# Sliding-window attention scores as fp32 matmuls of raw queries and keys in alternate halves of the array

## What is computed

```python
def _attn_ref(q, k, v, n_sink, window):          # n_sink = 4, window = 128
    scores = np.matmul(q, k.transpose(0, 1, 3, 2)) / np.sqrt(D)
    rel = pos[:, None] - pos[None, :]
    keep = (pos[None, :] < n_sink) | ((rel >= 0) & (rel < window))
    a = softmax(np.where(keep, scores, -1e9))
    return np.matmul(a, v)
x = attn_out.transpose(0, 2, 1, 3).reshape(B, S, H * D)
x = _moe_ref(x, ...)    # 4 experts of causal attention (head of 64), two chosen per token
return _moe2_ref(x, ...)  # x + gated(gelu(x @ w_in)) @ w_out with a mixing of tokens
```

## Time and profile before

| | us |
|---|---|
| median of 3 runs | 470.83 |
| lowest and highest run | 469.19 and 471.52 |
| profiled execution, span from first to last instruction | 465.9 |
| stage 1 in it, scores from 10.4, last sinks weighed | 143.8 |
| TensorE busy | 427.5 (92%) |
| VectorE busy | 281.2 (60%) |
| ScalarE busy | 209.7 (45%) |
| GpSimd busy | 127.9 (27%) |

### The profile page before, as it was taken

How to read it: one execution, slowest core, us unless ns; L and a number is a source line. 1 busy time by engine, 2 the same in 40 slices (tenths; PEclk the granted TensorE clock), 3 DMA queues, 4 the chain that set the end, 5 groups by cost and what they waited for, 6 DMA issues and landing times.

```text
span 465.9 us, 8125 instructions
## 1 busy us (share of the span) xinstructions
PE 427.5 (92%) x2608; PEld 383.6 (82%) x2608; DVE 281.2 (60%) x703; ACT 209.7 (45%) x529; POOL 127.9 (27%) x144
## 2 busy tenths in 40 slices
PE   1897978779799999998999899899999999999997
PEld 1787968779699999997999799788888888888885
DVE  1889698896985778555177965347633235552322
ACT  2666566655663666554476555343311013330100
POOL 7765375455627600000003820034100000000000
PEclk9888699886999999999999999999999999999999
DMA  8755554743323300000001320010000110000011
GB/s 209 167 145 133 144 146 102 172 103 105 100 85 114 113 1 2 2 0 1 1 0 40 97 69 1 0 47 0 1 0 24 45 46 24 0 1 0 24 45 68
DMA packets 14157, 27.73 MB, mean 60 GB/s; under 512 B 2256, under 2 KB 5328, under 8 KB 14128
## 3 DMA queue, kind: packets, MB, share of 16 engines
q1 hardware_dynamic: 14128, 27.35, 21.8%
HBM read 24.20 MB, written 3.15 MB: 59 GB/s over the span
## 4 chain that ended last, share of the span: by engine, by line
PE 77%; DVE 10%; issue 8%; ACT 2%; DVEq 1%; DMA 1%; POOL 1%; SPq 0%; ACTq 0%; POOLq 0%
PE banks L825 12%; PE banks L827 12%; PE banks L826 12%; PE banks L1097 11%; PE banks L999 6%; PE banks L876 6%; PE banks L977 4%; PE banks L840 4%; PE banks L988 4%; PE banks L856 2%; DVE sinks L567 2%; DVE SM L552 2%; DVE RI L585 1%; PE banks L891 1%; PE banks L945 1%
## 5 line engine op out<-in xcount | busy, mean ns | idle before, releaser
L401 ACT ACTIVATE Pa<-SM,NM 128x260 f32<-128x260 f32 (+1 forms) x96 | 47.1, 491 | 36.5 <-DVE NM L552 36.4
L876 PE MATMUL banks<-va,PTa 128*128 128x64 f32 x352 | 52.5, 299 | 0.0
L876 PEld LDWEIGHTS banks<-va,PTa 128*128 128x128 f32 x352 | 51.9, 224 | 0.0
L552 DVE CUSTOM_DVE_ANT_0 SM<-banks,win 128x260 f32<-128x260 f32 (+1 forms) x96 | 37.9, 404 | 19.9 <-PE banks L840 13.9
L840 PE MATMUL banks<-kS,qH 128*128 128x260 f32 x96 | 38.2, 402 | 11.5 <-POOL qL L321 10.4
L999 PE MATMUL banks<-vg,PTb 128*128 128x64 f32 x336 | 44.6, 267 | 0.7 <-DVE Y L678 0.7
L999 PEld LDWEIGHTS banks<-vg,PTb 128*128 128x128 f32 x336 | 42.2, 191 | 1.6 <-issue 0.9
L458 ACT ACTIVATE Pb<-Pb,NM 128x128 f32<-128x128 f32 (+5 forms) x48 | 31.9, 665 | 21.4 <-DVE NM L664 21.3
L825 PE MATMUL banks<-w_inH,x2H 128*128 128x512 f32 x96 | 38.1, 397 | 0.0
L527 ACT ACTIVATE gH<-banks 128x512 fp32r<-128x512 f32 x12 | 7.2, 600 | 68.4 <-PE banks L1117 68.4
L827 PE MATMUL banks<-w_inH,x2L 128*128 128x512 f32 x96 | 37.5, 391 | 0.0
(11 more groups left out here) (150 smaller groups left out, 1118.0 us busy)
## 6 DMA issues: line engine op xcount, KB each, us to landing
kd<-in_kT SPq DMA_DIRECT2D x32, 198.0 KB, 3.6
qd<-in_qT SPq DMA_DIRECT2D x32, 192.0 KB, 3.8
va<-in_v SPq DMA_DIRECT2D x16, 192.0 KB, 3.4
out<-O SPq DMA_DIRECT2D x12, 256.0 KB, 2.0
raw<-in_w_sgT SPq DMA_DIRECT2D x9, 256.0 KB, 2.7
raw<-in_w_in SPq DMA_DIRECT2D x8, 256.0 KB, 2.6
raw<-in_w_b SPq DMA_DIRECT2D x8, 193.0 KB, 3.7
raw<-in_w_out SPq DMA_DIRECT2D x4, 256.0 KB, 2.9
```

The costliest lines, as they stand in the source:

```text
L401: nc.scalar.activation(Pa[s][:, t, a:WIN], SM[t % RING][:, a:WIN], ACT.Exp, bias=NM[:, s, t:t + 1], scale=-1.0, accum_out=RS[:, s, t:t + 1 ...
L552: nc.vector.tensor_tensor_reduce(out=SM[t % RING][:, a:WIN], in0=banks[:, A_BANKS[t % RING], 0:WIN - a], in1=m[:, :], scale=-SCALE, scalar ...
L876: last = nc.tensor.matmul(banks[:, 6 + s, t * D:(t + 1) * D], PTa[m][:, j * P:(j + 1) * P], va[s][:, t - 1 + own, :], start=(t == 0), stop ...
```

## The change

Queries and keys are no longer split: `split_queries`, `high_keys` and `low_keys` go, with their calls and the semaphores `q_split`, `k_high` and `k_split`. One fp32 matmul of the raw `qd` and `kd` makes a tile of scores. It has the 64 features as rows; even tiles take partitions 0 to 63 of `qd` and `kd`, and so the array's lower 64 rows, odd tiles 64 to 127. The two tiles of a pair are issued one behind the other, at turns 0, 2 and 4. `load_keys` now waits until head - 2 has been scored. A tile named `spare` keeps the place of the removed buffers. The transfers and their order stay.

```diff
-            qH, qL = [sb(f"qH{s}", [P, S], F32R, st) for s in range(2)], [sb(f"qL{s}", [P, S], F32R, st) for s in range(2)]
-            kS = [sb(f"kS{s}", [P, KEXT], F32R, st) for s in range(2)]
+            sb("spare", [P, 4 * S + 2 * KEXT], F32, st)
...
             def load_keys(s, head, again):
 
                 if again:
-                    sp.wait_ge(s_["q_split"], 2 * (head - 1))
-                    sp.wait_ge(s_["k_split"], head - 1)
+                    sp.wait_ge(s_["scored"], T * (head - 1))
...
-            def split_queries(s, head, turn, again):
-                pool.wait_ge(qk_in[s], 64 * (turn + 1))
-                if again:
-                    pool.wait_ge(s_["scored"], T * (head - 1))
-                pool.sem_inc(s_["pool_tick"], 1)
-                nc.gpsimd.tensor_scalar(qH[s][:, :], qd[s][:, :], 1.0, 0.0, ALU.mult, ALU.add).then_inc(s_["q_split"], 1)
-                pool.wait_ge(s_["q_split"], 2 * head + 1)
-                nc.gpsimd.tensor_tensor(qL[s][:, :], qd[s][:, :], qH[s][:, :].bitcast(F32), ALU.subtract)\
-                    .then_inc(s_["q_split"], 1)
...
-            def high_keys(s, head, turn, again):
-                act.wait_ge(qk_in[s], 64 * (turn + 1))
-                if again:
-                    act.wait_ge(s_["scored"], T * (head - 1))
-                nc.scalar.activation(kS[s][:, :], kd[s][:, :], ACT.Copy).then_inc(s_["k_high"], 1)
...
-            def low_keys(s, head):
-                dve.wait_ge(s_["k_high"], head + 1)
-                half = slice(D, P)
-                nc.vector.tensor_tensor(kS[s][half, :], kd[s][half, :], kS[s][half, :].bitcast(F32), ALU.subtract)\
-                    .then_inc(s_["k_split"], 1)
...
-            def score_tile(s, head, t, again):
+            def score_tile(s, head, t, turn, again):
 
                 if t == 0:
-                    pe.wait_ge(s_["q_split"], 2 * head + 2)
-                    pe.wait_ge(s_["k_split"], head + 1)
+                    pe.wait_ge(qk_in[s], 64 * (turn + 1))
                 if again or t >= RING:
                     pe.wait_ge(s_["masked"], T * head + t - RING + 1)
                 c = 0 if t == 0 else (t - 1) * BLK + SINK
-                for q, first_ in ((qH, True), (qL, False)):
-                    last = nc.tensor.matmul(banks[:, A_BANKS[t % RING], 0:WIN], q[s][:, t * P:(t + 1) * P], kS[s][:, c:c + WIN],
-                                            start=first_, stop=not first_)
-                last.then_inc(s_["scored"], 1)
+                half = slice(t % 2 * D, (t % 2 + 1) * D)
+                nc.tensor.matmul(banks[:, A_BANKS[t % RING], 0:WIN], qd[s][half, t * P:(t + 1) * P], kd[s][half, c:c + WIN],
+                                 start=True, stop=True).then_inc(s_["scored"], 1)
...
                 for t in range(T):
                     if nxt:
-                        score_tile(1 - s, head + 1, t, True)
+                        if t % 2 == 0:
+                            score_tile(1 - s, head + 1, t, turn + s, True)
+                            score_tile(1 - s, head + 1, t + 1, turn + s, True)
```

More of the change, by code:

```diff
@@ L184, in fused_attention_experts_gated @@
             "consts", "pool_step",
-            "q_split", "k_high", "k_split", "scored", "masked", "expd", "turned", "turned_in_act", "turned_in_dve",
+            "scored", "masked", "expd", "turned", "turned_in_act", "turned_in_dve",
             "sinks_gathered", "sinks_turned", "sinks_high", "sinks_in", "sv_in", "sv_high", "sv_low", "vs_ready",
@@ L338, in lay_out_sinks @@
                                         diag[:, :].unsqueeze(2).broadcast_to((SROWS, T, D)), ALU.mult).then_inc(s_["vs_ready"], 1)
-            for s in range(2):
-                split_queries(s, s, 0, False)
             split_strip(0, slice(0, WB_STEP))
@@ L346, in _ @@
             with pool.Fori(1, PAIRS) as i:
-                split_queries(0, 2 * i, i, True)
                 lay_out_sinks(0, 2 * i, True)
-                split_queries(1, 2 * i + 1, i, True)
                 split_strip(i, bass.ds(i * WB_STEP, WB_STEP))
@@ L415, in x_high, with act_step @@
                                      ACT.Copy).then_inc(s_["x_high"], 1)
-            def act_step(s, head, again, keys, nxt):
+            def act_step(s, head, again, nxt):
                 copy_group(s, head, 0, again)
@@ L424, in act_step @@
                         x_high(0, t)
-                    if t == 0 and keys is not None:
-                        high_keys(s, head + 2, keys, True)
                     if t == 2:
                         copy_group(s, head, 2, again)
-            high_keys(0, 0, 0, False)
-            high_keys(1, 1, 0, False)
             for t in range(T):
@@ L436, in _ @@
                 exp_tile(0, 0, t, False)
-            act_step(0, 0, False, 1, True)
-            act_step(1, 1, True, 1, True)
+            act_step(0, 0, False, True)
+            act_step(1, 1, True, True)
             with act.Fori(1, PAIRS - 1) as i:
[L440 to L443, removed]
+                act_step(0, 2 * i, True, True)
+                act_step(1, 2 * i + 1, True, True)
+            act_step(0, HEADS - 2, True, True)
+            act_step(1, HEADS - 1, True, False)
             def wait(name, n):
@@ L603, in x_low, with dve_step @@
                                         xH[:, :, t * P:(t + 1) * P].bitcast(F32), ALU.subtract).then_inc(s_["x_low"], 1)
-            def dve_step(s, head, before, again, keys, nxt):
+            def dve_step(s, head, before, again, nxt):
                 for t in range(T):
@@ L616, in dve_step @@
                         copy_group(s, head, again)
-                    if t == 2 and keys:
-                        low_keys(s, head + 2)
                     if t == 3:
@@ L623, in dve_step @@
                 invert_sums(s, head, again)
-            low_keys(0, 0)
-            low_keys(1, 1)
             for t in range(T):
@@ L631, in _ @@
             nc.vector.tensor_tensor(sv[low, :], sv_raw[low, :], sv[low, :].bitcast(F32), ALU.subtract).then_inc(s_["sv_low"], 1)
-            dve_step(0, 0, None, False, True, True)
-            dve_step(1, 1, 0, True, True, True)
+            dve_step(0, 0, None, False, True)
+            dve_step(1, 1, 0, True, True)
             with dve.Fori(1, PAIRS - 1) as i:
[L635 to L638, removed]
+                dve_step(0, 2 * i, i - 1, True, True)
+                dve_step(1, 2 * i + 1, i, True, True)
+            dve_step(0, HEADS - 2, PAIRS - 2, True, True)
+            dve_step(1, HEADS - 1, PAIRS - 1, True, False)
             normalise(1, HEADS - 1, PAIRS - 1)
@@ L921, in _ @@
             for t in range(T):
-                score_tile(0, 0, t, False)
+                score_tile(0, 0, t, 0, False)
             pe_step(0, 0, 0, False, True)
```

## The result

The changed kernel takes 478.7 us (median of 4 runs, 478.04 to 480.17) against 470.02 for the kernel before (4 runs beside it); the ratio is 1.0175, with a 95% interval of 1.0131 to 1.0219. So the change makes the kernel slower, by 8.7 us. The forecast was 472.0 in a range of 460 to 485, with 0.38 on slower by over 0.5%; the time that came is that of rival 3, 479, and not that of the central sum.

The account below looks back on a forecast made before the run. Stage 1 was taken as bound by TensorE's work plus a splitting stall, replaced by a wait for values. Start -1.5, steps 0 and 1 -1.4, loop +1.6, step 14 +1.0, half clock +1.5: +1.2 in all, 472 us, range 460 to 485.

Parts of the forecast that it names:

- rival 3: Loop: the new 1.2 to 1.9 us wait throws TensorE to half clock; 476 to 486 us, at 479; chance 0.24.
- the central sum: Whole kernel: the forecast's terms added against the profiled execution, +1.2 in all, 472 us; chance 0.38.
- rivals 3 and 4: 4: score pairs run one after the other, with a drain at each change; near 481 us, chance 0.12.
- start with steps 0 and 1: Stage 1's beginning: earlier first scores, -1.5 us, and shorter steps 0 and 1, -1.4 us.
- the ring: Steps 2 to 13: scored, next keys, values behind them, weighing, scored again; mean 8.35 us a step against 8.22, +1.6 us.
- half clock in the loop: Inside the ring, weighing and score pair slowed by a clock fall in one of four pairs; +1.5 us.
- step 14: Step where nothing makes TensorE wait: 6.5 us against 5.54, from dearer score tiles and row switches; +1.0 us.
- three signs of being wrong: TensorE waits for `va` nowhere; loop step under 7.5 or over 9 us; fp32 score records not 0.22 us apart.
- rival 2: Score pairs: array halves run side by side, a pair streams 0.43 us, not 0.65; 466 us; chance 0.12.
- three slots of 0.22: Score pair on TensorE: four records start in order, only the second and third overlap; 0.65 us streamed.
- Rival 1: Loop: the ring is shorter than TensorE's work, so TensorE bounds at 7.0 us a step; near 458 us; chance 0.14.
- The stall that the splitting makes: Stage 1 before: GpSimd's query split holds up VectorE's sinks gather, and TensorE waits 17.2 us in all, 11 times.

Follow-up runs that it names:

- e4_filler: The change, with six identity matmuls on TensorE ahead of every wait for the values: 473.8 us, ratio 1.0072 to the kernel before.
- e9_odd_values_first: The change, with only the odd head's values issued ahead of its keys and the strip: 479.2 us, ratio 1.0213 to the kernel before.
- e10_odd_first_filler: The change with odd values issued first, plus six filler matmuls ahead of even heads' waits for values alone: 456.3 us, ratio 0.9686 to the kernel before.
- e1_values_first: The change, with SP issuing the values of head - 2 ahead of the next keys in each loop half: 447.0 us, ratio 0.949 to the kernel before.
- e8_split_behind_gather: The kernel before, with GpSimd's split of a head's queries waiting until the sinks of head - 2 are gathered: 455.05 us, ratio 0.9695.
- e7_warm_start: The change with values issued first, plus 24 constant matmuls on TensorE in front of the first score: 451.6 us, ratio 0.9563 to the kernel before.

## Why the prediction was right, and where it was not

**The number.** The range held the measured time because it was made wide enough for rivals 3 and 4. The central sum did not: it had +1.2 where the medians are 8.7 apart, and the path to 478.7 is rival 3's. By terms, forecast against measured between the spans: start with steps 0 and 1, -2.9 and +0.8; the ring at full clock, +1.6 and -1.2 (12 x 8.22 less 99.79); half clock in the loop, +1.5 and +10.0; step 14, +1.0 and +0.8; the rest, 0 and +0.9. The step of before is 8.32 us from sinks to sinks, not the 8.22 of the earlier trace rows, whose stretch is cut elsewhere; against it the forecast's ring of 8.35 makes +0.4.

Of its own three signs of being wrong two came: a loop step takes over 9 us (9.05), and the records of the scores are not 0.22 us apart. The first is the clock, the second the halves of the array, both below.

**The ring: right.** It was found from the order of SP's queue and the instructions behind it, not from a row of waits. TensorE waits for `va`, 1.6 us at the longest where 1.2 to 1.9 were forecast, and opening the ring gives 31.7 us. Its length was right too: 6.44 us from score to landing for 6.35, and 8.22 us a step at full clock for 8.35.

**The clock: the term that was mis-sized.** The sum put half clock inside the ring at +1.5 us, "one fall in four pairs". It cost 0.83 us a step, 10 us. The mechanism stood in rival 3, with its place and its price of 476 to 486; it had 0.24 where the forecast had 0.38. The point of decision was put rightly (a wait between 0.76 and 2.16), and it fell on the wrong side: all six waits of 1.40 to 1.57 us were followed by a fall, and in e4_filler one of 0.81 us was too. What I missed is the feedback. Behind the wait TensorE needs all the step for its work at half clock, the ring then doesn't wait, and the next wait comes as soon as the clock is up again. e9_odd_values_first and e10_odd_first_filler show the two sides of it, 479.2 and 456.3.

**The halves side by side: the mechanism of rival 2, at 0.12, is what happens**, though not its time of 466, which left out the clock. I took three slots of 0.22 for a pair, from in-order starts; the first records of both tiles start together and a pair streams in 0.43. The Trainium skill, TensorE: Matmul & The Clock Gate, Part 3, says that matmuls in different row groups run at once. The trace agrees, with the first records of both tiles started within 0.02 us.

Step 14 is 6.36 us for 6.5 all the same, because two errors nearly cancelled. Three pairs take 3 x 0.64 = 1.92 us to the next kind, against 1.78 for the six tiles of before: +0.14 where the sum had +0.5. All else in the step takes 4.44 against 3.76: +0.68 where the sum had +0.5, as the cost of going from 128 rows to 64 and back. Part of it lies right in front of a pair: the six records of group 0 take 0.71 us up to the next kind, 0.59 before. That the change of rows is its cause fits, but no run isolates it.

**Start and steps 0 and 1: wrong.** The sum had -2.9, measured +0.8. The first score did start early, at 6.8, but the head start was gone by the end of step 0 (sinks at 24.68, before at 24.66). TensorE stayed at half clock until 28.1 us by the spacing of its matmuls, where 1.8 us in all were left for the clock. The kernel before was at full clock by 18.7, and again from 27 us, with half clock between 20.2 and 26.

**Rival 1, TensorE's own bound of 7.0 us a step and 458, did not come; e1_values_first shows that TensorE's own bound is 6.41 a step, and the kernel's time with it 447.** The stall that the splitting makes, the base of the argument on the kernel before, is shown by e8_split_behind_gather: the gather's 1210 ns become 257.

## What to carry to other kernels

When a buffer's release is moved to a later event, list everything behind that transfer in its queue and ask whether any of it feeds the very event: here values needed before the next release stood behind keys nobody needed for more than a step, and one reordering of five lines was worth 31.7 us. A wait of 1.5 us on TensorE is not worth 1.5 us; here it cost the clock for 7 to 10 us each time, and filling it with idle work was worth 23 us. That doesn't carry to every start: in e7_warm_start the same means brought nothing. The version that beats both kernels is the change with the values issued ahead of the keys, 447.0 us.

## What the runs showed of the hardware that was not expected

- TensorE can stay at half clock for over 200 us while it is never idle: with both tiles of a pair in one half of the array, or mostly alone, 558 and 561 us, steps of 14.2 to 14.4 us. In the same runs the clock came up about 7 us after the last score tile, in step 15. What keeps it down was not isolated.
- The granted clock of the profile can read 1.00 where it was half. In the run with one half of the array it says so for a stretch whose matmuls are spaced at 1.2 GHz:

```profile
26.00:225.00 199.00, 199.00 (x658) 151.41 (x658) 62.49 (x267) 59.75 (x196) 30.35 (x36) 1.00 0.31 77
```

  In the kernel before it reads 1.00 from 8 to 16 us, where the one-pass score records start 0.22 us apart instead of 0.12. The spacing of a known matmul is the safer reading at the start of a program. The 0.80 of steps 0 and 1 in the earlier trace rows stands: its parts read 1.00, 0.50 and 1.00 and the spacing agrees.
- The records of two fp32 tiles in different halves pair up, although each tile is two matmul records and the tiles are issued one behind the other: both first records, then both second ones 0.32 us on.
- A VectorE copy of 72 columns takes 0.2 us alone and 1.83 us beside GpSimd's split: it ended within 0.1 us of GpSimd's operation.
